# Expert layer of a three-part kernel: the expert with the most tokens so far is put first, its weights are loaded late in the attention, and the zero rows are written in two groups

## The reference, cut to what matters

```python
B, H, S, D = 4, 8, 576, 64                 # attention, then N = 2304 tokens of 512
x = attention(q, k, v, M_prev, z_prev, beta)          # float32
e_idx = argmax(x @ w_gate, axis=1)                    # one of E = 8 experts
for e in range(E):
    m = e_idx == e
    out[m] = gate_w[m] * eom[m, e] * (relu(x[m] @ w1[e]) @ w2[e])   # 512 -> 1024 -> 512
h = out @ w_in;  result = (h - tanh(h)) @ w_out       # 512 -> 2048 -> 512
```

## Time and profile before

| | |
|---|---|
| median of 3 runs | 1030.22 us (1030.07 to 1033.31) |
| profiled execution | 1030.83 us, its span 1029.0 us |
| mean granted clock of TensorE | 0.988 |
| busy share of the span | PE 97%, PEld 79%, DVE 63%, ACT 49%, POOL 46% |
| chain that ended last | PE 77%, DVE 6%, POOL 2%, issue 1% |
| experts' products | L1381 to L1383 and L1394 to L1396, 200 of each, 391 to 406 ns |
| POOL's split of a half unit (L537) | 30 of 4613 ns |

### The profile page before, as it was taken

How to read it: one execution, slowest core, us unless ns; L and a number is a source line. 1 busy time by engine, 2 the same in 40 slices (tenths; PEclk the granted TensorE clock), 3 DMA queues, 4 the chain that set the end, 5 groups by cost and what they waited for, 6 DMA issues and landing times.

```text
span 1029.0 us, 16805 instructions
## 1 busy us (share of the span) xinstructions
PE 996.1 (97%) x5482; PEld 817.5 (79%) x5483; DVE 645.9 (63%) x1241; ACT 503.6 (49%) x1045; POOL 474.0 (46%) x334
## 2 busy tenths in 40 slices
PE   7999989899889999999999999999999999999998
PEld 4667758576547888888888879999999999999997
DVE  3777776877634444444444448777777777777664
ACT  6877777686235120022112047555555555655654
POOL 6665586775489833057537137332232322322221
PEclk9999999999889999999999999999999999999999
DMA  9555665431477443146482211010010010100001
GB/s 210 137 162 151 178 198 165 130 103 39 145 280 284 141 138 123 46 167 220 143 302 106 71 41 32 1 32 32 1 62 1 19 44 1 37 26 1 32 1 31
DMA packets 51009, 103.66 MB, mean 101 GB/s; under 512 B 7424, under 2 KB 16640, under 8 KB 50432
## 3 DMA queue, kind: packets, MB, share of 16 engines
q1 hardware_dynamic: 34416, 56.68, 19.0%
q10 hardware_dynamic: 13616, 36.70, 9.8%
q0 software_dynamic: 2912, 9.44, 3.0%
HBM read 82.62 MB, written 20.19 MB: 100 GB/s over the span
## 4 chain that ended last, share of the span: by engine, by line
PE 77%; DVE 6%; POOL 2%; issue 1%; ACTq 1%; ACT 0%; DVEq 0%
PE scores L1440 6%; PE scores L1442 6%; PE scores L1441 6%; PE scores L1381 5%; PE scores L1383 5%; PE scores L1382 5%; PE average L1396 4%; PE average L1395 4%; PE average L1394 4%; PE average L1272 2%; PE average L1457 2%; PE mix L1458 2%; PE turned L1457 2%; PE average L1458 2%; PE turned L1458 2%; PE mix L1457 2%
## 5 line engine op out<-in xcount | busy, mean ns | idle before, releaser
L574 POOL TENSOR_TENSOR g_lo<-g,g_hi 128x384 fp32r<-128x384 f32 x96 | 97.9, 1019 | 274.9 <-ACT g_hi L778 274.3
L537 POOL TENSOR_TENSOR ring<-ring 128x2048 fp32r<-128x2048 f32 x30 | 137.4, 4613 | 106.2 <-ACT ring L717 102.3
L717 ACT ACTIVATE ring<-ring 128x2048 fp32r<-128x2048 f32 x30 | 55.7, 1907 | 180.1 <-PE scores L1383 81.7
L1440 PE MATMUL scores<-yt_hi,w_in_hi 128*128 128x384 f32 x384 | 130.9, 341 | 1.7 <-DVE yt_lo L1131 1.7
L1442 PE MATMUL scores<-yt_hi,w_in_lo 128*128 128x384 f32 x384 | 129.2, 337 | 0.0
L1441 PE MATMUL scores<-yt_lo,w_in_hi 128*128 128x384 f32 x384 | 128.8, 335 | 0.0
L768 ACT ACTIVATE sq<-scores 128x384 f32<-128x384 f32 x96 | 47.2, 491 | 163.8 <-PE scores L1442 163.8
L1123 DVE COPY_PREDICATED ser<-big,th 128x384 f32<-128x384 int32 x96 | 118.9, 1239 | 3.3
L1118 DVE TENSOR_TENSOR ser<-ser,sq 128x384 f32<-128x384 f32 x96 | 55.9, 582 | 95.8 <-ACT ser L771 92.0
L600 ACT ACTIVATE prob<-scores,nmx 128x128 f32<-128x128 f32 (+3 forms) x128 | 66.4, 525 | 43.8 <-DVE nmx L853 40.8
L1381 PE MATMUL scores<-ring,xt_hi 128*128 x200 | 81.1, 406 | 3.1 <-POOL ring L537 1.7
(11 more groups left out here) (255 smaller groups left out, 2505.4 us busy)
## 6 DMA issues: line engine op xcount, KB each, us to landing
ring<-in_w ACTq DMA_DIRECT2D x13, 2048.0 KB, 9.0
q_sb<-in_qt SPq DMA_DIRECT2D x48, 288.0 KB, 4.2
k_sb<-in_kt SPq DMA_DIRECT2D x32, 288.0 KB, 4.3
xin<-x_sorted SPq DMA_DIRECT2D x27, 256.0 KB, 2.8
y_sorted<-y_sb SPq DMA_DIRECT2D x25, 256.0 KB, 2.1
v_sb<-in_v SPq DMA_DIRECT2D x16, 256.0 KB, 2.8
ring<-in_w SPq DMA_DIRECT2D x8, 512.0 KB, 4.1
w_out_sb<-in_w_out ACTq DMA_DIRECT2D x1, 4096.0 KB, 16.2
```

Source lines behind the costliest of these rows:

```text
L537: pool.tensor_tensor(ring[:, ring_at(k), 1, part], ring[:, ring_at(k), 1, part].bitcast(F32), ring[:, ring_at(k), 0, part].bitcast(F32), A ...
L574: pool.tensor_tensor(g_lo[:, t % GRING, :], g32[:, t % 2, :], g_hi[:, t % GRING, :].bitcast(F32), ALU.subtract).then_inc(g_lo_ok, 1)
L1440: mm(ff_h(t), w_h, yt_hi[:, j % 2, c, :], start=c == 0, stop=False)
```

## The change

It does these things:

- When two batches are counted (`CHOICE = 1`), DVE finds the expert with the most tokens so far (`largest`, in pair 11) and makes an order of the experts in which this one and expert 0 have changed places (`order`, in pair 12, `r_order`). Everything behind (slots, weights, the table) goes by that order.
- SP waits for `r_order` in its turn for pair 11 and loads the first expert's two units there and in its turn for pair 12, instead of expert 0's an eighth per pair from pair 3 on. Both units are split in sixteenths in pairs 14 to 16 (`HIGH`, `LOW_AHEAD`, `LOW_BEHIND`), the last four low parts on POOL behind the scatters.
- The first 128 rows of the first expert are loaded as soon as the last scores are done, ahead of the last batch's routing; PE transposes them between its logits (`turn_in(0, 0, o_ps[1])`), and `first_up` follows the last count at once. The 60 idle products are gone. `first_down` follows with `down`'s products of slot 0, which came in slot 1 before.
- SP writes the zeros of the first two experts ahead of the second and third rows, waiting for these two, for the scatters and for the table's third row (`r_slots`, new); the other six (three by SP, three by ACT) come behind these two loads, and the fourth rows wait for them.
- Slots 0 to 6 are written out, slots 7 to 24 are a loop. DVE's `swap` (four small operations) is added to the table, and once more to the row numbers at its end.

The diff, cut to its core:

```diff
+HIGH = {(14, 0): (0,), (14, 1): (1,), (14, 2): (2,), (14, 3): (3,), (15, 0): (4, 5), (15, 1): (6, 7), (15, 2): (8,), (15, 3): (9,),
+        (15, 4): (10,), (16, 0): (11, 12), (16, 1): (13, 14), (16, 2): (15,)}
+LOW_AHEAD = {14: (0,), 15: (3, 4, 5, 6, 7, 8), 16: (9, 10, 11)}
+LOW_BEHIND = {14: (1, 2)}
...
+        def expert_of(queue, k):
+            return queue.value_load(order_i[0:1, k // 2:k // 2 + 1], min_val=0, max_val=E - 1)
+        def fill(queue, j, done):
+            e = expert_of(queue, 2 * j)
+            row = queue.value_load(fill_i[0:1, bass.ds(e, 1)], min_val=0, max_val=E * REG)
+            queue.dma_start(xs[bass.ds(row, P), :], zeros[:, :]).then_inc(done, 16)
...
     # SP
-                if 3 <= n < 3 + 2 * CD:
-                    load_first_expert(n - 3)
+                if n in (11, 12):
+                    if n == 11:
+                        sp.wait_ge(r_order, 1)
+                    first = sp.value_load(order_i[0:1, 0:1], min_val=0, max_val=E - 1)
+                    for c in range(CD):
+                        load_first_expert((n - 11) * CD + c, first)
+            row = sp.value_load(first_i[0:1, 0:1], min_val=0, max_val=E * REG)
+            sp.wait_ge(q_split, NP)
+            sp.wait_ge(scored, NP * QT)
+            sp.dma_start(xin[:, 0, :], xs[bass.ds(row, P), :]).then_inc(xin_ok[0], 16)
             sp.wait_ge(x_ok, NP * QT)
-            load_unit(sp, 2)
+            load_unit(sp, 2, expert_of(sp, 2))
             sp.wait_ge(r_fill, 1)
-            for e in range(0, E, 2):
-                fill(sp, e)
+            for j in range(2):
+                fill(sp, j, first_filled)
             sp.wait_ge(zero_out, 16 * (SLOTS - N // P + 1))
+            sp.wait_ge(first_filled, 32)
             sp.wait_ge(scattered, 16 * TILES)
-            sp.wait_ge(filled, 16 * E)
-            sp.wait_ge(r_table, 1)
+            sp.wait_ge(r_slots, 1)
-            for k in range(XIN):
+            for k in range(1, XIN):
                 load_x(k, k)
+            for j in range(2, E, 2):
+                fill(sp, j, filled)
+            sp.wait_ge(filled, 16 * (E - 2))
     # POOL, behind the attention
-                if n == NP:
-                    for i in range(2, QT):
-                        scatter(B - 2, i)
+            for i in range(2, QT):
+                scatter(B - 2, i)
             for i in range(QT):
                 scatter(B - 1, i)
+            pool.wait_ge(r_slots, 1)
+            for q in range(12, SIXTEENTHS):
+                early_low(q)
             pool.wait_ge(r_tails, 1)
-            for k in range(1, UNITS):
+            for k in range(2, UNITS):
     # ACT
+                if q == 8:
+                    act.wait_ge(k_split, NP)
+                    act.wait_ge(q_split, NP)
-            act.wait_ge(r_fill, 1)
-            for e in range(1, E, 2):
-                fill(act, e)
-            for k in range(1, 3):
-                convert(k)
+            convert(2)
             act.wait_ge(scattered, 16 * TILES)
-            act.wait_ge(xin_ok[0], 16)
+            act.wait_ge(xin_ok[1], 16)
+            for j in range(3, E, 2):
+                fill(act, j, filled)
     # DVE
+            def largest():
+                rs(dve.tensor_reduce(first_s[:, 0:1], n_first[:, :], AX.X, ALU.max))
+                rs(dve.tensor_scalar(n_first[:, :], n_first[:, :], first_s[:, 0:1], None, ALU.is_equal))
+                rs(dve.tensor_tensor(n_first[:, :], n_first[:, :], desc[:, :], ALU.mult))
+                rs(dve.tensor_reduce(first_s[:, 1:2], n_first[:, :], AX.X, ALU.max))
+            # order(): seven operations of 8 columns, four of them waited for, then r_order
+            # swap(): four operations of 8 columns, each waited for
             gates_of(0, B - 1)
+            split_x(0, o_ps[1])
             take_logits(B - 1, t_ps[1], 0)
...
+            dve.tensor_tensor(table[:, 2, :], row0, spare, ALU.subtract).then_inc(r_slots, 1)
+            relu(0)
+            split_hid(0)
             # the rest of the table, r_table
+            split_x(1, t_ps[0])
             # gates of the last batch, swap, row numbers, r_tails
     # PE
+                if i == 2:
+                    turn_in(0, 0, o_ps[1])
             count(B - 1, t_ps[0], 0, QT + 1)
-            idle_products(s_ps[1][1], AT_EXPERTS)
-            pe.wait_ge(r_table, 1)
+            first_up(up_at)          # as up(0), without the table: waits xt_ok 1, part_lo 2
+            turn_hid(0)
+            idle_products(s_ps[0][0], AT_LAST)
+            first_down(down_at)      # waits ht_ok 2, part_lo 3, at its middle turn_in(0, 1) and part_lo 4
+            pe.wait_ge(r_table, 1)
+            up(1)
+            turn_in(0, 2, t_ps[0])
+            turn_hid(1)
+            for t in range(2, PEELED):
+                slot(t, t, (t + 1) // XIN)
```

More of the change, by code:

```diff
@@ L29 @@
 RING = 5
[L30 removed]
+SIXTEENTHS = 16
+CHOICE = 1
+AT_START, AT_LAST = 36, 9
 XIN = 3
@@ L973, in _ @@
                     if 0 <= b < B - 1 and i == 2 and half == 3:
-                        place_rows(b, m_ps, RANKS)
+                        place_rows(b, m_ps, LOGITS if b == CHOICE else RANKS)
+                    if b == CHOICE and half == 3 and i == 4:
+                        largest()
+                    if b == CHOICE + 1 and half == 0 and i == 1:
+                        order()
                     if i == 0 and n >= 2:
@@ new lines, in _, with swap @@
+            dve.sem_inc(r_fill, 1)
+            n_e, slots_e, end_e, start_e, gap_o, n_o, part_e, step_e = (small_e[:, r, :] for r in range(8))
+            def swap(to, values):
+                rs(dve.tensor_tensor(part_e, values, chosen[:, :], ALU.mult))
+                rs(dve.tensor_tensor(to, values, part_e, ALU.subtract))
+                rs(dve.scalar_tensor_tensor(to, chosen[:, :], values[:, 0:1], to, ALU.mult, ALU.add))
+                rs(dve.tensor_reduce(to[:, 0:1], part_e, AX.X, ALU.add))
@@ new lines, in _ @@
+            dve.tensor_tensor(started[:, :, :], start_e[:, None, :].to_broadcast(wide),
+                              slot_f[:, :, None].to_broadcast(wide), ALU.is_le)
+            rs(dve.scalar_tensor_tensor(gap_o, start_e, -float(P), base_o[:, :], ALU.mult, ALU.add))
+            dve.tensor_copy(step_e[:, 0:1], gap_o[:, 0:1])
+            rs(dve.tensor_tensor(step_e[:, 1:E], gap_o[:, 1:E], gap_o[:, 0:E - 1], ALU.subtract))
+            begun, row0, unused, spare, from3, from4, from6, from8 = (small_t[:, r, :] for r in range(8))
@@ new lines, in _ @@
+            rs(dve.scalar_tensor_tensor(from6, begun, -2.0, from6, ALU.mult, ALU.add))
+            dve.scalar_tensor_tensor(table[:, 1, :], from6, RING + 1.0, from4, ALU.add, ALU.add)
+            dve.scalar_tensor_tensor(table[:, 3, :], from6, float(RING), from3, ALU.add, ALU.add)
+            dve.tensor_scalar(table[:, 0, :], begun, -1.0, None, ALU.add)
+            dve.tensor_scalar(ups[:, :], end_e, 2.0, None, ALU.mult)
+            dve.tensor_scalar(ends[:, :], end_e, 1.0, None, ALU.add).then_inc(r_table, 1)
@@ new lines, in _ @@
+            split_x(1, t_ps[0])
+            dve.wait_ge(r_exp, 4)
+            gates_of(B - 1, B)
+            wide = [P, TILES, E]
+            swap(n_e, gap_o)
+            rs(dve.tensor_tensor(hot2[:, :, :], hot[:, 1:TILES + 1, :], n_e[:, None, :].to_broadcast(wide), ALU.mult))
+            rs(dve.tensor_reduce(row_f[:, 1, :], hot2[:, :, :], AX.X, ALU.add))
+            rs(dve.tensor_tensor(y_u[:, :], row_f[:, 0, :], row_f[:, 1, :], ALU.subtract))
+            for b in range(0, B, 2):
+                a, z = b * QT + QT - 1, (b + 1) * QT + QT - 1
+                dve.tensor_copy(y_u[D:P, a:a + 1], y_u[0:D, z:z + 1])
+                last = dve.tensor_copy(gate[D:P, a:a + 1], gate[0:D, z:z + 1])
@@ new lines, in _, with slot @@
+            rs(last)
+            dve.sem_inc(r_tails, 1)
+            def slot(t, at, half):
+                relu(t)
+                split_x(t + 1, t_ps[0])
+                copy_y(t - 1, half, at - 1)
+                split_hid(t)
+            copy_y(0, 0, 0)
+            relu(1)
+            split_x(2, t_ps[0])
+            split_hid(1)
+            for t in range(2, PEELED):
+                slot(t, t, (t - 1) // 2)
+            with dve.Fori(0, (SLOTS - PEELED) // SPAN) as i:
+                for at in range(PEELED, PEELED + SPAN):
+                    slot(i * SPAN + at, at, i * (SPAN // 2) + (at - 1) // 2)
@@ L1356, in _, with turn_in @@
                         turn_x(b * QT + 4, s_ps[m % 2][1])
+            def turn_in(round, k, bank):
+                pe.wait_ge(xin_ok[k % XIN], round * 16 + 16)
+                for c in range(CD):
+                    last = pe.transpose(bank[:, c * P:(c + 1) * P], xin[:, k % XIN, c * P:(c + 1) * P], ident[:, :])
+                last.then_inc(x_turned, 1)
             for i in range(QT):
```

228 lines of the change are left out of this document (118 added, 110 removed).

## The result

The changed kernel takes 1034.49 us (median of 20 runs, 1032.13 to 1039.45), the kernel before beside it 1031.16 (20 runs, 1029.01 to 1033.31): a ratio of 1.0032, 95% interval 1.0024 to 1.0041. It is slower by some 3.3 us. The forecast was 1025.9, which is 4.3 us less than before. The profiled execution took 1033.03 us, with a span of 1031.2 and a granted clock of 0.983.

What follows compares the result with a forecast made beforehand. PE bounds the experts' stage; ahead of it some 20 us are a chain through other engines. Head -16.8, attention +2.5, hole +9.9 sum to -4.4: profiled 1030.8 to 1026.4, median 1025.9, range 1015.5 to 1030.5 us.

Steps and rivals of the forecast that it cites:

- the attention: Added work in the attention's pairs: 2.5 us slower, between -1 and 4.4.
- the hole: Slot 18, eighth expert: PE stands 7.8 us for unit 14, then 2.1 at half clock; cost 9.9 us.
- the head: Start of the experts' stage: `up(2)` starts at 305.5 instead of 322.26, a gain of 16.8 us.
- Queries behind the order: SP's queue: queries behind the order and 2 MB of loads land at 215 to 216.5, wanted 215.5; 0 to 1 us.
- ACT's in pair 14: ACT's high parts ahead of the split of keys and queries: about two on the path, 1.0 to 1.3 us.
- POOL's six of pair 15: Six low parts on POOL take 7.5 us, to 258.9, when its next work came at 258.83: free.
- `largest` and `order`: DVE's added operations in pairs 11 and 12: 0.9 and about 1.2 us.
- The 2.1: Behind the wait at slot 18, PE begins at half the clock: 7.7 - 5.6 = 2.1 us more.
- The fourth: Rival: SP's wait for the order starves pairs 13 and 14 of queries, +10 to +16, 1036 to 1042 us; chance 0.08.
- The first: Rival: no hole at slot 18, by a sooner load or unseen cover; 1016.0 us; chance 0.10.
- The second: Rival: second or fourth rows or low parts late, or attention at its upper bound; 3 us more, 1029; chance 0.17.
- The third: Rival: `first_down` and `up(1)` at half clock, 2.1 us each, up to 4.2; 1028 to 1030 us; chance 0.10.

Runs made afterwards that it cites:

- Two experiments: Changed kernel with the first expert's loads one pair later, 1030.78 us; changed kernel with the order of experts made in pair 11, 1031.97 us.
- second execution: The changed kernel profiled once more, with no edit: 1035.18 us, span 1033.3.
- The experiment on the kernel before: Kernel before, with POOL's low part of pair 14 moved behind that pair's queries: 1031.39 us, ratio 1.0005 to the kernel before.
- The experiment with the first four experts: Changed kernel, with the first expert chosen among experts 0 to 3 only: 1023.18 us, ratio 0.993 to the kernel before.
- the parted kernel: Changed kernel, with three of POOL's six low parts left in pair 15 and later ones shifted into the head: 1032.7 us, ratio 1.0025 to the kernel before.

## Why the prediction was wrong

The profiled execution was forecast at 1026.4 and took 1033.0. Of these 6.6 us the attention makes 4.6, the hole 1.1, and 1.2 lie ahead of pair 12; the head was 0.3 better than forecast.

**The attention is the step that failed**: "I take 2.5", with an upper bound of 4.4. Measured, it is 7.1 and 9.2 in pairs 12 to 15. Two terms were put at nothing that were not: DVE's small operations standing beside POOL's long ones, and the lower clock behind a new wait in the attention. By its parts, in the first execution:

- Queries behind the order: "0 to 1". Measured 2.3 (4.0 in the second). The prediction had the order at about 206.5, the landing at 215 to 216.5. The order was done at 208.7, and the landing came at 219.8. Of the 3.3 us beyond 216.5, 2.2 are `order` standing behind POOL. SP's part was right, 3.0 us from the order to the issue of the queries at 211.66. The rest is the landing, 8.1 us behind the 2 MB, where the prediction left 5.5 to 7. The second execution's further 1.7 us are the clock. Two experiments remove ACT's wait in different ways, by 2.5 and 3.7 us of the whole time.
- "ACT's in pair 14 ... about two, 1.0 to 1.3": the pair lost 2.4, but not to ACT. All of it is in three operations of the pick that stand beside POOL: 0.5 us beside its split of the queries, 1.9 beside its low parts. The experiment on the kernel before shows that mechanism alone.
- "POOL's six of pair 15 ... free": 1.7 us. I asked when POOL's own next work came, and that was right; I did not ask who can't run beside it.
- `largest` and `order`, 0.9 and 1.2: pair 12 lost 0.7 (1.2 in the second execution), in line.
- The rows for this were there. In the trace of the kernel before, the cast of the row numbers takes 0.17 us at the shortest, 1.23 in the median and 2.30 at the longest, and the longest stands beside 2.65 us of POOL. I read the means of groups and did not compare a small operation with itself.

```profile
L944 DVE CAST row_u<-row_f x4: 170/1231/2297, 125.9 to 279.8; 128x5 uint32<-128x5 f32 x4
```

**The head** was right: 17.1 against 16.8. Its first step began later with the attention; the steps are 7.6 (forecast 7.7), 4.2 (3.5), 6.05 (6.05), 5.4 (5.6) and 2.5 (3.0). The second rows were there in time, with little over: they landed at 301.2 and were wanted at 302.4. Without the two groups it would have been 7 us worse.

**The hole at slot 18** was right: 7.7 against 7.8. What follows it cost 3.3 where 2.1 were set. The 2.1 came from a slot whose products ran at the lower level for some 4.5 us; here the windows show it for some 5.4, from 518.6 to about 524, and `up(19)` follows `up(18)` by 14.9 us instead of 12.3, which is 2.6 of the 3.3. Another 0.4 lies between `up(2)` and `up(3)`, far ahead of the hole; the last 0.3 were not traced. The experiment with the first four experts puts the whole hole at 11, as the trace does.

**The balance.** Here the head is counted from the last maximum of pair 15 to `up(2)`, and "hole" is all from there to the last slot. First profiled executions: pairs 12 to 15 +7.1, head -17.0, hole +11.0, and 1.2 that the changed kernel is late ahead of pair 12, together 2.3; the spans differ by 2.2. Second ones: +9.2, -17.3, +11.4, and this time the kernel before is 2.2 late ahead of pair 12, together 1.1; the spans differ by 1.0. Without what lies ahead of pair 12, which is spread, the change itself makes +1.1 in the one and +3.3 in the other; the medians, 3.3 apart, agree with the second. The two differ mostly in pair 13, 18.6 and 20.3 us, by the clock. Over the 20 runs of the changed kernel the time goes with the mean granted clock in the same sense: the four at 0.983 or 0.984 took 1033.0 to 1034.2 us, the ten at 0.975 to 0.979 took 1033.8 to 1039.5. Where in each of them the clock fell is not shown, since only the first has a trace.

**The rivals.** The fourth, that SP's wait for the order starves the attention, had its place right and its price too high (that ACT waits for queries in pair 12 or 13 was also named as a sign of being wrong): ACT did wait for queries, at the end of pair 12, for 3.6 us, not for 5 to 8 in two pairs. It was to decide "from 7.5 us in all", and the attention's 7.1 to 9.2 us are about that point, but more than half of the 7.1 come from DVE beside POOL (2.4 in pair 14 and 1.7 in pair 15, without the order's delay), which no rival had. The first would have been right with another order. The second did not happen as stated, apart from its words on the attention's upper bound, which was passed; no rows came late. The third did not happen in the two places that it named: the granted clock is 0.99 to 1.00 in every 2 us from 292 to 314, through `first_down` and `up(1)`, with transposes and the waits for DVE between them. It fell behind the new wait in the attention instead, where no term stood for it.

## What to carry to other kernels

Before work is put into an engine's idle time, look at what the other engines do in that time that shares something with it: here long operations of POOL held up DVE's small ones, which stood on the critical chain. The mark of it in a profile is a small operation whose longest instance is many times its shortest. And a change of order at one end of a ring moves the deadlines at the other end: here the hole took back 11.0 of the head's 17.1 us, and choosing the first expert among the first four removed it. Last, where a new wait makes TensorE stand, price it twice, with the clock kept and with the clock at its lower level behind it: the same 3.6 us wait cost 2.3 us in one execution and 4.0 in another.

## What the runs showed of the hardware

- Some DVE operations from SBUF to SBUF stand until POOL's running operation is done: 128x5, 128x8 and 128x40, 0.17 to 0.20 us alone, took 0.72 to 2.66 beside POOL's `TENSOR_TENSOR` of 1.25 to 2.7 us. In the parted kernel one stood over the rest of one part and all of the next. Operations of one column (0.15 at 206.16), `TENSOR_REDUCE` of 40 columns (0.19 at 248.34, with POOL busy from 246.97 to 249.47) and those that read PSUM (L978, 0.20 at 262.19) went through. The Trainium skill ("SBUF — State Buffer", Who interferes with whom) has a shared port pair, an exclusive lock that DVE's operations with two SBUF inputs need beside a GpSimd operation that reads SBUF, and its casts and `TENSOR_SCALAR` in a two-port mode too, and `TENSOR_REDUCE` never; the second to issue stands until the first is done. The traces agree in each of these forms; the one-column operations that went through are a `TENSOR_SCALAR` too.
- Behind like waits of TensorE the granted clock fell in some executions and stayed in others: behind ACT's wait for queries (3.6 and 3.7 us) it was 1.00 in the changed kernel's first execution and 0.57 in its second, with PE busy for 1.78 and 1.67 of the 4 us ahead. Pair 13 was 1.7 us longer in the second.
- 288 KB of queries issued right behind 2 MB on SP's queue landed 8.1 us after their issue.
- Zero writes whose row is read through a register cost SP's queue 1.4 to 1.5 us each with two register loads (two in 2.90 us, three in 4.25, changed kernel), and 2.05 each where SP and ACT wrote four each at one time (8.20 and 9.65 us). In the kernel before, with one register load each, the same four and four took 6.28 and 5.29. Why they were slower with two loads and two queues was not tested: SP's three and ACT's three of the changed kernel overlap for 2.3 us and show no such price on SP. All eight together cost the head 7 us, and not the 1.5 to 3 expected.
